# Other slots for the second element's spectra and for layer 2's weight sums in a two-layer kernel behind a Fourier filter

## The chip, the cores and the metric

The kernel runs on one core of a Trainium2 chip. The metric is the device time of one execution in microseconds, taken as the median of several runs. One further execution was profiled; all rows below come from it.

## What is computed

Each of two batch elements (3008 tokens of 256 channels) is filtered in the frequency domain, and the 6016 tokens then go through two feed-forward layers of width 2048. All of it is float32.

```
X = np.fft.rfft(x, axis=1)
y = np.fft.irfft(X * (filt_r + 1j * filt_i), n=3008, axis=1)
h = y.reshape(6016, 256) @ w_in
g = np.maximum(h, 0.0) + alpha * np.minimum(h, 0.0)
z = g @ w_out
h2 = np.maximum(z @ w2_in, 0.0)
out = (h2 * h2) @ w2_out
```

## The kernel before

The five engines each run a program written out by hand; semaphores join them, and each engine takes its instructions in the order in which they stand. TensorE (PE) does the matrix products, ScalarE (ACT) and VectorE (DVE) read PSUM, GpSimd (POOL) helps with SBUF to SBUF work, and SyncE (SP) issues nearly all DMAs.

A float32 product is made of three fast ones: each operand is cut into a high part (rounded) and a low part (the rest), and high by high, low by high and high by low are summed.

The first element's transform comes first, alone. Then runs a loop over **slots**, `n = 0 .. 191`. The tokens are cut into 12 groups of 500 or 504, and the hidden units into 8 pairs of 128-wide tiles, so a slot is one pair `p = n % 8` of one group `g = n // 8`; slots 0 to 95 are layer 1, the others layer 2. In slot n:

- PE runs `up(n)` (12 matmuls in two halves `j`, into one PSUM bank each), then `down_high(n - 2)` and `down_low(n - 2)` (21 matmuls of 250 columns: seven products in place of eight, by a Strassen scheme). In slots with `p = 2` the low part is put off to the middle of the next `up`.
- ACT writes the two ReLUs, `g_raw`, and later the high part `g_hi` of the slot before (L606).
- DVE turns each half into the activation with one operation (L913; both are one name, `g_raw`, and each adds one to `g_ready`), makes two sums (L923), and then `g_low(n - 1)`, the low part `g_lo` (L898). With `p = 1` the outputs of the group before are put together (`combine`, L883 to L892) and `g_low` is put off, so that DVE runs two of them in the slot with `p = 2`.
- POOL makes two more sums (L594, L597), after which ACT can write `g_hi`.

`up(n + 1)` of half j waits until DVE has done L913 of slot n, half j (`g_ready`), since it writes over the bank.

Into slots 0 to 95 work of two other kinds is put, by tables of slot numbers.

- **The second element's transform.** It has 12 units u. In slot `B_SLOT[u]` PE makes the spectrum (L1028 to L1031, three matmuls of 512 columns, `spectrum_1`) at the end of its slot; ACT swaps its halves (`swapped`) at the start of the next slot; DVE multiplies with the filter at the end of its own slot `B_SLOT[u]` (L805 `product_re`, and four pieces L812 `product_im`); POOL adds the two in the next slot (L560). Two slots on, ACT and POOL split the result into `y_hi` and `y_lo`, and four slots on (`V_LAG`) PE does the inverse (`inverse_1`, the same lines L1028 to L1031, before a spectrum that has the same slot). The product lives in one of two buffers, `slot = n % f.deep` with `deep` 2, and so unit u waits for the inverse of unit u - 2:

```
dve.wait_ge(f.v_done, free(n, f.deep))
```

- **Sums of layer 2's weights.** For each of the 8 pairs q, a load is issued in slot `W2_SLOT[q]`; in the next slot DVE makes four sums of 128x128 tiles (`sums`, L822 to L829) as the last thing of its slot; ACT (`s_hi`), POOL (`s_lo`, in three parts, three to five slots on) and two stores to HBM follow.

In slots with `p = 5` PE also makes the next group's input from the first element's or the second's transform (`y_group`, L1080), and waits there for the DVE products of all spectra that stand in slots before.

Of the kernel before, what the change touches and what calls it, by code (L numbers as in the profile page):

```python
# [75 lines left out]
AHEAD_BANK = (2, 3, 0, 1)  # L76
AHEAD_PART = (1, AHEAD_A - 2, AHEAD_A)
A_SLOT = [None] * AHEAD_A + [0, 1, 2, 2, 3, 3, 4, 4]
B_SLOT = [12, 14, 16, 20, 22, 24, 28, 30, 32, 34, 36, 38]
V_LAG = 4  # L80
CONST_SLOT = 7
VC_P, Y_P, IN_P = 3, 5, 6
LATE_W = 5
W2_SLOT = [45, 51, 57, 63, 69, 75, 81, 88]
W2_LOW = ((3, 0, 4), (4, 4, 8), (5, 8, W_T))

WARM_COLS, WARM_X = 2 * P, 8
# [98 lines left out]
def spectral_mix_two_ffn(nc, x, filt, w1, w2, alpha, sign, consts, consts_1, consts_full, const_y, out):  # L186
# [7 lines left out]
    with ctx:  # L194
# [95 lines left out]
        def _(sp):  # L290
# [50 lines left out]
            def load_filter(f, n, slot):  # L341
                if f is f1 or n >= f.filters:
                    sp.wait_ge(f.im_ready, free(n, f.filters))

                for c in ((n % 2,) if f is f0 else (0, 1)):
                    sp.dma_start(f.filt[c * N2:(c + 1) * N2, slot, :], filt[n * N2:(n + 1) * N2, :]
                                 ).then_inc(f.filt_loaded[slot], 16)

            def store_v(f, half, m, slot):
                sp.wait_ge(f.v_ready, done(half * B_HALF + m))  # L350
                sp.dma_start(v_rows[f.batch].rearrange("(p k) d -> p k d", k=K1)
                             [:, m * WIDE:(m + 1) * WIDE, half * P:(half + 1) * P],
                             f.v_out[:, slot, :].rearrange("p (k d) -> p k d", k=WIDE)
                             ).then_inc(f.v_stored[slot], 16)
# [86 lines left out]
            for n in range(2 * SLOTS_1):  # L441
# [6 lines left out]
                if n < SLOTS_1:  # L448
# [9 lines left out]
                    for u in range(B_UNITS):  # L458
                        if B_SLOT[u] - 3 == n:
                            if u == 0:  # L460
# [4 lines left out]
                    for u in range(B_UNITS):  # L465
                        if B_SLOT[u] - 1 == n:
                            load_filter(f1, u, u % f1.filters)
                    for u in range(B_UNITS):
                        if B_SLOT[u] + V_LAG + 1 == n:
                            store_v(f1, *divmod(u, B_HALF), u % f1.vs)  # L470
# [5 lines left out]
                for q in range(FP):  # L476
                    if W2_SLOT[q] + 6 == n:
                        cols = slice(q * W_T * P, (q + 1) * W_T * P)
# [6 lines left out]
                for q in range(FP):  # L485
                    if W2_SLOT[q] == n:
                        if q > 0:
# [40 lines left out]
        def _(pool):  # L528
# [27 lines left out]
            def add(n):  # L556
                slot = n % f1.deep
                pool.wait_ge(f1.re_ready, done(n))
                pool.wait_ge(f1.im_ready, done(n))
                pool.tensor_tensor(f1.y_re[:, slot, :], f1.y_re[:, slot, :], f1.y_im[:, slot, :],  # L560
                                   ALU.add).then_inc(f1.y_ready, 1)
# [4 lines left out]
            for n in range(2 * SLOTS_1):  # L566
                r, h = n % RING, HALF[n // FP % GROUPS]

                if n < SLOTS_1:
                    for u in range(B_UNITS):  # L570
                        if B_SLOT[u] + 1 == n:
                            add(u)
                    for u in range(B_UNITS):
                        if B_SLOT[u] - 1 == n:
                            pool.wait_ge(f1.t_hi_ready, u + 1)
                            low(f1.t_lo[:, u % f1.raw, :], f1.t_raw[:, u % f1.raw, :], f1.t_hi[:, u % f1.raw, :],
                                f1.t_lo_ready)
                        if B_SLOT[u] + 2 == n:
                            pool.wait_ge(f1.y_hi_ready, u + 1)
                            low(f1.y_lo[:, u % f1.deep, :], f1.y_re[:, u % f1.deep, :], f1.y_hi[:, u % f1.deep, :],  # L580
                                f1.y_lo_ready)
                    for q in range(FP):
                        for at, a, b in W2_LOW:
                            if W2_SLOT[q] + at == n:
                                pool.wait_ge(s_hi_ready, q + 1)
# [15 lines left out]
        def _(act):  # L601
# [100 lines left out]
            for n in range(2 * SLOTS_1):  # L702
# [54 lines left out]
                for q in range(FP):  # L757
                    if W2_SLOT[q] + 2 == n:
                        act.wait_ge(s_sums_ready, q + 1)
# [12 lines left out]
        def _(dve):  # L772
# [46 lines left out]
            def sums(raw, loaded, need, signal, at):  # L819

                dve.wait_ge(loaded, need)
                dve.scalar_tensor_tensor(out=raw[:, S1N, :], in0=raw[:, A21, :], scalar=-1.0, in1=raw[:, A22, :],  # L822
                                         op0=ALU.mult, op1=ALU.subtract).then_inc(signal[1], 1)
                dve.wait_ge(signal[1], 3 * at + 1)
                dve.scalar_tensor_tensor(out=raw[:, S2, :], in0=raw[:, S1N, :], scalar=-1.0, in1=raw[:, A11, :],
                                         op0=ALU.mult, op1=ALU.subtract).then_inc(signal[1], 1)
                dve.tensor_tensor(raw[:, S3, :], raw[:, A11, :], raw[:, A21, :], ALU.subtract).then_inc(signal[1], 1)
                dve.wait_ge(signal[1], 3 * at + 3)
                dve.tensor_tensor(raw[:, S4, :], raw[:, A12, :], raw[:, S2, :], ALU.subtract).then_inc(signal[0], 1)  # L829
# [72 lines left out]
            for n in range(2 * SLOTS_1):  # L902
# [43 lines left out]
                for q in range(FP):  # L946
                    if W2_SLOT[q] + 1 == n:
                        sums(s_raw, s_loaded, 16 * q + 16, (s_sums_ready, s_sum_step), q)
# [362 lines left out]
```

## Time and profile before

| what | value |
|---|---|
| median of 3 runs | 1121.08 us (1120.23 to 1121.08) |
| the profiled execution: its time, and its span from first to last instruction | 1121.51 us, 1119.7 us |
| PE busy | 1111.2 us, 99% |
| DVE busy | 961.2 us, 86% |
| ACT busy | 662.5 us, 59% |
| POOL busy | 650.4 us, 58% |
| share of PE in the chain that ended last | 88% (DVE 4%, all else 2% and less each) |
| the slots 0 to 95 | from 66.52 us to 614.73 us |

Busy time is the union of an engine's instructions. A matmul's end is modelled and overlaps the start of the next one, so the length of a slot is best read from the start of its first matmul (L1102) to that of the next slot's.

### The profile page before, as it was taken

Reading aid. Unit: us, or ns where it says so; the run is one execution under the profiler, and the core shown is the slowest. Engines: PE = TensorE matmul, PEld = TensorE weight load, DVE = VectorE, ACT = ScalarE, POOL = GpSimd, SP = SyncE. Lnnn points to the kernel's source line nnn. Section 1 sums busy time; section 2 is a strip of 40 time slices with the busy share of each in tenths; the row PEclk is TensorE's granted clock in tenths of the full one; section 3 lists DMA queues with packets and bytes.
Section 4 is the critical chain, followed back from the end, with each engine's and each line's share of the span. In section 5 each row is a group of like instructions: output and inputs, shape, how many; then the busy total and the mean of one; then the engine's idle time right before and its main releaser. Section 6 shows DMA issues by size and latency. Waiting matters only on the chain.

```text
span 1119.7 us, 17393 instructions
## 1 busy us (share of the span) xinstructions
PE 1111.2 (99%) x6997; PEld 992.1 (89%) x6997; DVE 961.2 (86%) x1099; ACT 662.5 (59%) x785; POOL 650.4 (58%) x479
## 2 busy tenths in 40 slices
PE   9999999999999999999999999999999999999998
PEld 8568999898999989999898999999999999999997
DVE  4748899989988998898988888888898898888887
ACT  4956566766655555555555565555556555555653
POOL 0837587777856567666657455455455555555453
PEclk9999999999999999999999999999999999999999
DMA  9973225144120431312318600110110110110100
GB/s 213 276 222 85 68 67 134 34 111 133 40 78 1 137 97 59 110 49 89 110 60 297 228 23 14 38 34 4 37 37 1 37 38 1 38 38 1 38 19 19
DMA packets 56408, 87.24 MB, mean 78 GB/s; under 512 B 4712, under 2 KB 44168, under 8 KB 56328
## 3 DMA queue, kind: packets, MB, share of 16 engines
q1 hardware_dynamic: 56128, 85.98, 26.2%
q8 instruction: 55, 0.90, 0.3%
q14 instruction: 25, 0.20, 0.1%
q10 hardware_dynamic: 200, 0.15, 0.0%
HBM read 52.82 MB, written 33.29 MB: 77 GB/s over the span
## 4 chain that ended last, share of the span: by engine, by line
PE 88%; DVE 4%; DMA 2%; ACT 2%; issue 1%; POOL 1%; SPq 1%; DVEq 0%; ACTq 0%; POOLq 0%
PE bank L1102 15%; PE bank L1107 15%; PE bank L1103 14%; PE bank L1141 13%; PE bank L1128 13%; PE bank L1130 13%; PE bank L1080 3%; DMA filt_b<-filt 2%; DVE g_lo L898 1%; DVE g_raw L913 1%; PE bank L1000 1%; ACT filt_b L606 1%; PE bank L994 1%; DMA vc<-v_rows 0%; ACT t_hi_b L606 0%
## 5 line engine op out<-in xcount | busy, mean ns | idle before, releaser
L594 POOL TENSOR_TENSOR g_raw<-g_raw 128x250 f32<-128x250 f32 (+1 forms) x191 | 280.9, 1471 | 393.4 <-DVE g_raw L923 393.4
L898 DVE TENSOR_TENSOR g_lo<-g_raw,g_hi 128x1750 fp32r<-128x1750 f32 (+1 forms) x191 | 424.0, 2220 | 45.1 <-ACT g_hi L606 44.4
L732 ACT ACTIVATE g_raw<-bank 128x500 f32<-128x500 f32 (+1 forms) x384 | 226.2, 591 | 320.5 <-PE bank L1107 280.9
L606 ACT ACTIVATE g_hi<-g_raw 128x1750 fp32r<-128x1750 f32 (+1 forms) x191 | 318.9, 1670 | 50.4 <-POOL g_raw L597 48.8
L1130 PE MATMUL bank<-g_hi,w_lo 128*128 128x250 f32 (+1 forms) x1337 | 320.0, 279 | 0.0
L1128 PE MATMUL bank<-g_hi,w_hi 128*128 128x250 f32 (+1 forms) x1337 | 319.5, 279 | 0.0
L1102 PE MATMUL bank<-in_hi,w_hi 128*128 128x500 f32 (+1 forms) x768 | 302.3, 394 | 2.0 <-DVE g_raw L913 2.0
L1103 PE MATMUL bank<-in_hi,w_lo 128*128 128x500 f32 (+1 forms) x768 | 298.3, 388 | 0.0
L1130 PEld LDWEIGHTS bank<-g_hi,w_lo 128*128 128x128 f32 x1337 | 252.8, 189 | 7.5
L1128 PEld LDWEIGHTS bank<-g_hi,w_hi 128*128 128x128 f32 x1337 | 252.5, 189 | 7.4
L597 POOL TENSOR_TENSOR g_raw<-g_raw 128x250 f32<-128x250 f32 (+1 forms) x191 | 247.8, 1297 | 15.0
L1107 PE MATMUL bank<-in_lo,w_hi 128*128 128x500 f32 (+1 forms) x768 | 236.8, 390 | 0.0
L1141 PE MATMUL bank<-g_lo,w_hi 128*128 128x250 f32 (+1 forms) x1337 | 187.7, 280 | 0.3
L1141 PEld LDWEIGHTS bank<-g_lo,w_hi 128*128 128x128 f32 x1337 | 171.3, 189 | 3.5 <-DVE g_lo L898 2.0
L1107 PEld LDWEIGHTS bank<-in_lo,w_hi 128*128 128x128 f32 x768 | 144.4, 188 | 30.1
L1102 PEld LDWEIGHTS bank<-in_hi,w_hi 128*128 128x128 f32 x768 | 144.6, 188 | 25.8 <-DVE g_raw L913 2.6
L1103 PEld LDWEIGHTS bank<-in_hi,w_lo 128*128 128x128 f32 x768 | 144.5, 188 | 23.5 <-issue 1.4
L913 DVE SCALAR_TENSOR_TENSOR g_raw<-g_raw,rest_sb,bank 128x500 f32<-128x500 f32 (+1 forms) x192 | 135.9, 729 | 33.1 <-ACT g_raw L732 33.1
L916 DVE TENSOR_TENSOR g_raw<-g_raw,bank 128x500 f32<-128x500 f32 (+1 forms) x192 | 127.7, 670 | 33.0 <-ACT g_raw L732 31.9
L923 DVE TENSOR_TENSOR g_raw<-g_raw 128x500 f32<-128x500 f32 (+1 forms) x192 | 135.5, 706 | 6.6
L1080 PEld LDWEIGHTS bank<-const_y_sb,vc 96*128 96x128 f32 x288 | 33.2, 192 | 1.7 <-DMA vc<-v_rows 1.6
L1080 PE MATMUL bank<-const_y_sb,vc 96*128 96x94 f32 (+4 forms) x288 | 33.7, 273 | 0.2 <-DMA vc<-v_rows 0.2
(87 smaller groups left out, 612.7 us busy)
## 6 DMA issues: line engine op xcount, KB each, us to landing
filt_b<-filt SPq DMA_DIRECT2D x36, 256.0 KB, 4.6
vc<-v_rows SPq DMA_DIRECT2D x22, 288.0 KB
v_rows<-v_out_b SPq DMA_DIRECT2D x24, 256.0 KB, 4.5
w_rows<-s_hi SPq DMA_DIRECT2D x8, 704.0 KB, 5.3
w_rows<-s_lo SPq DMA_DIRECT2D x8, 704.0 KB, 3.5
w_hi<-w_rows SPq DMA_DIRECT2D x8, 704.0 KB, 5.4
w_lo<-w_rows SPq DMA_DIRECT2D x8, 704.0 KB, 7.6
w_raw<-w SPq DMA_DIRECT2D x8, 512.0 KB, 8.7
```

The costliest lines, as they stand in the source:

```text
L594: pool.tensor_tensor(g_raw[:, r, T2, 0:h], g_raw[:, r, B22, 0:h], g_raw[:, r, T1N, 0:h], ALU.add).then_inc(t2_ready, 1)
L597: pool.tensor_tensor(g_raw[:, r, T4, 0:h], g_raw[:, r, B21, 0:h], g_raw[:, r, T2, 0:h], ALU.subtract).then_inc(t4_ready, 1)
L606: return act.activation(dst, src, ACT.Copy)
L732: act.activation(g_raw[:, r, 2 * j:2 * j + 2, 0:h], h_ps[j][:, 0:2 * h].rearrange("p (j d) -> p j d", j=2), ACT.Relu, scale=-1.0 if n < SL ...
L898: dve.tensor_tensor(g_lo[:, q, B11:T4 + 1, 0:h], g_raw[:, q, B11:T4 + 1, 0:h], g_hi[:, q, :, 0:h], ALU.subtract).then_inc(g_lo_ready, 1)
L913: dve.scalar_tensor_tensor(out=piece, in0=piece, scalar=rest_sb[:, f:f + 1], in1=hidden, op0=ALU.mult, op1=ALU.add).then_inc(g_ready, 1)
L1102: pe.matmul(o, w_hi[:, p, 2 * j + k, :], in_hi[:, g % 2, k, cols], start=(k == 0), stop=False)
L1103: pe.matmul(o, w_lo[:, p, 2 * j + k, :], in_hi[:, g % 2, k, cols], start=False, stop=False)
L1107: mm = pe.matmul(o, w_hi[:, p, 2 * j + k, :], in_lo[:, g % 2, k, cols], start=False, stop=(k == KD - 1))
L1128: pe.matmul(o, w_hi[:, p, tile, :], g_hi[:, q, piece - B11, 0:h], start=(first and side == 0), stop=False, skip_group_check=True)
L1130: pe.matmul(o, w_lo[:, p, tile, :], g_hi[:, q, piece - B11, 0:h], start=False, stop=False, skip_group_check=True)
L1141: mm = pe.matmul(o, w_hi[:, p, tile, :], g_lo[:, q, piece, 0:h], start=False, stop=last, skip_group_check=True)
```

## The change

Two tables of slot numbers get other values; nothing else is touched.

```diff
-B_SLOT = [12, 14, 16, 20, 22, 24, 28, 30, 32, 34, 36, 38]
+B_SLOT = [11, 12, 14, 16, 19, 20, 22, 24, 27, 28, 30, 32]
...
-W2_SLOT = [45, 51, 57, 63, 69, 75, 81, 88]
+W2_SLOT = [39, 46, 52, 58, 66, 74, 82, 88]
```

The spectra stood three to a group (p = 4, 6, 0) and at last at p = 2, 4, 6; they now stand four to a group, at p = 3, 4, 6, 0. The sums, one slot after `W2_SLOT`, stood at p = 6, 4, 2, 0, 6, 4, 2, 1 and now stand at p = 0, 7, 5, 3, 3, 3, 3, 1. The inverses, four slots after the spectra, stood in slots 16, 18, 20, 24, 26, 28, 32, 34, 36, 38, 40, 42 and now stand in 15, 16, 18, 20, 23, 24, 26, 28, 31, 32, 34, 36.

On PE, the first inverse before the change, at the end of slot 16, with unit 2's spectrum behind it (`L1028` with `y_hi` is an inverse, with `t_hi` a spectrum):

```order
L1141 MATMUL bank<-g_lo,w_hi 128x250 [waits g_lo_ready]
L1141 MATMUL bank<-g_lo,w_hi 128x250 x6
L1028 MATMUL bank<-y_hi_b,const_b 128x512 [waits y_hi_ready_b1,v_ready_b1,in_lo_ready]
L1029 MATMUL bank<-y_hi_b,const_b 128x512
L1031 MATMUL bank<-y_lo_b,const_b 128x512 [waits y_lo_ready_b1]
L1028 MATMUL bank<-t_hi_b,const_b 128x512 [waits t_hi_ready_b1,im_ready_b1,const_ready_b1,in_lo_ready]
L1029 MATMUL bank<-t_hi_b,const_b 128x512
L1031 MATMUL bank<-t_lo_b,const_b 128x512 [waits t_lo_ready_b1]
```

And the first inverse after the change, at the end of slot 15, with the first matmul of slot 16 behind it:

```order
L1141 MATMUL bank<-g_lo,w_hi 128x250 [waits g_lo_ready]
L1141 MATMUL bank<-g_lo,w_hi 128x250 x6
L1028 MATMUL bank<-y_hi_b,const_b 128x512 [waits y_hi_ready_b1,v_ready_b1,in_lo_ready]
L1029 MATMUL bank<-y_hi_b,const_b 128x512
L1031 MATMUL bank<-y_lo_b,const_b 128x512 [waits y_lo_ready_b1]
L1102 MATMUL bank<-in_hi,w_hi 128x500 [waits in_hi_ready,g_ready]
```

The inverse has moved up by one slot, and unit 2's spectrum by two, from the end of slot 16 to that of slot 14.

On DVE, the end of slot 14 and the start of slot 15, which read alike in both kernels but for their unit: before, the product (L805, L812) is that of unit 1; after the change it is that of unit 2, and its wait for `v_done_b1` is the one for unit 0's inverse. These are the rows after the change:

```order
L923 TENSOR_TENSOR g_raw<-g_raw 128x2x250 [waits g_ready]
L898 TENSOR_TENSOR g_lo<-g_raw,g_hi 128x7x250 [waits g_hi_ready]
L805 TENSOR_TENSOR y_re_b<-bank,filt_b 128x512 [waits filt_loaded0_b1,v_done_b1,swap_ready_b1,spec_done_b1]
L812 SCALAR_TENSOR_TENSOR y_im_b<-swapped_b,sign_sb,filt_b 128x128 x4
L913 SCALAR_TENSOR_TENSOR g_raw<-g_raw,rest_sb,bank 128x2x250 [waits relu_ready] x2
L923 TENSOR_TENSOR g_raw<-g_raw 128x2x250 [waits g_ready]
```

What moved is which unit stands there: slots 11 and 12 now hold units 0 and 1.

On DVE, slots 58 and 59 (p = 2 and 3) before the change, with the weight sums between them:

```order
L898 TENSOR_TENSOR g_lo<-g_raw,g_hi 128x7x250 [waits g_hi_ready]
L822 SCALAR_TENSOR_TENSOR s_raw<-s_raw 128x128 [waits s_loaded]
L825 SCALAR_TENSOR_TENSOR s_raw<-s_raw 128x128 [waits s_sum_step]
L827 TENSOR_TENSOR s_raw<-s_raw 128x128
L829 TENSOR_TENSOR s_raw<-s_raw 128x128 [waits s_sum_step]
L913 SCALAR_TENSOR_TENSOR g_raw<-g_raw,rest_sb,bank 128x2x250 [waits relu_ready] x2
```

And the same place after the change:

```order
L898 TENSOR_TENSOR g_lo<-g_raw,g_hi 128x7x250 [waits g_hi_ready]
L913 SCALAR_TENSOR_TENSOR g_raw<-g_raw,rest_sb,bank 128x2x250 [waits relu_ready] x2
L923 TENSOR_TENSOR g_raw<-g_raw 128x2x250 [waits g_ready]
L898 TENSOR_TENSOR g_lo<-g_raw,g_hi 128x7x250 [waits g_hi_ready]
L822 SCALAR_TENSOR_TENSOR s_raw<-s_raw 128x128 [waits s_loaded]
L825 SCALAR_TENSOR_TENSOR s_raw<-s_raw 128x128 [waits s_sum_step]
```

The sums have moved from the end of slot 58 to that of slot 59.

## Rows read from the trace of the kernel before

**Rows 1.** The page: the span, busy time, the granted PE clock by slices.

```profile
span 1119.7 us, 17393 instructions
...
PE 1111.2 (99%) x6997; PEld 992.1 (89%) x6997; DVE 961.2 (86%) x1099; ACT 662.5 (59%) x785; POOL 650.4 (58%) x479
...
PEclk9999999999999999999999999999999999999999
```

**Rows 2.** Waits of PE and its weight loads: us in total, times, longest.

```profile
PE bank L1102 <- DVE g_raw L913: 2.0, 3, 1.2
...
PEld bank L1141 <- DVE g_lo L898: 2.0, 6, 0.6
```

**Rows 3.** Timeline of PE, first matmuls of slots: start us, us, instruction, [idle before].

```profile
127.77 0.39 PE L1102 MATMUL bank<-in_hi,w_hi 128*128 128x500 f32 x1
...
133.78 0.39 PE L1102 MATMUL bank<-in_hi,w_hi 128*128 128x500 f32 x1
...
139.62 0.40 PE L1102 MATMUL bank<-in_hi,w_hi 128*128 128x500 f32 x1
...
153.07 0.39 PE L1031 MATMUL bank<-t_lo_b,const_b 128*128 128x512 f32 x1
153.29 0.39 PE L1102 MATMUL bank<-in_hi,w_hi 128*128 128x500 f32 x1
...
158.44 0.39 PE L1102 MATMUL bank<-in_hi,w_hi 128*128 128x500 f32 x1
...
165.00 0.39 PE L1102 MATMUL bank<-in_hi,w_hi 128*128 128x500 f32 x1
...
170.15 0.40 PE L1102 MATMUL bank<-in_hi,w_hi 128*128 128x500 f32 x1
...
272.32 0.39 PE L1102 MATMUL bank<-in_hi,w_hi 128*128 128x500 f32 x1
...
279.62 0.49 PE L1102 MATMUL bank<-in_hi,w_hi 128*128 128x500 f32 x1 [1.15 <-DVE g_raw L913]
...
416.65 0.50 PE L1102 MATMUL bank<-in_hi,w_hi 128*128 128x500 f32 x1 [0.42 <-DVE g_raw L913]
```

**Rows 4.** The chain that ended last, at the end of slot 35: start us, us, what.

```profile
277.40 1.52 DVE y_im_b L812 x4
278.92 0.66 DVE g_raw L913
```

**Rows 5.** Timeline of DVE, slots 12 to 17.

```profile
137.20 1.37 DVE L913 SCALAR_TENSOR_TENSOR g_raw<-g_raw,rest_sb,bank 128x500 f32<-128x500 f32 x2
...
141.86 0.68 DVE L805 TENSOR_TENSOR y_re_b<-bank,filt_b 128x512 f32<-128x512 f32 x1
142.46 1.12 DVE L812 SCALAR_TENSOR_TENSOR y_im_b<-swapped_b,sign_sb,filt_b 128x128 f32<-128x128 f32 x4
143.51 1.36 DVE L913 SCALAR_TENSOR_TENSOR g_raw<-g_raw,rest_sb,bank 128x500 f32<-128x500 f32 x2
...
154.79 0.69 DVE L805 TENSOR_TENSOR y_re_b<-bank,filt_b 128x512 f32<-128x512 f32 x1
155.40 1.61 DVE L812 SCALAR_TENSOR_TENSOR y_im_b<-swapped_b,sign_sb,filt_b 128x128 f32<-128x128 f32 x4
156.93 1.37 DVE L913 SCALAR_TENSOR_TENSOR g_raw<-g_raw,rest_sb,bank 128x500 f32<-128x500 f32 x2
...
165.14 2.56 DVE L898 TENSOR_TENSOR g_lo<-g_raw,g_hi 128x1750 fp32r<-128x1750 f32 x1 [1.14 <-ACT g_hi L606]
...
169.27 1.37 DVE L913 SCALAR_TENSOR_TENSOR g_raw<-g_raw,rest_sb,bank 128x500 f32<-128x500 f32 x2
```

**Rows 6.** Timeline of ACT, the swap behind a spectrum.

```profile
153.49 1.21 ACT L606 ACTIVATE swapped_b<-bank 64x512 f32<-64x512 f32 x2 [0.47 <-PE bank L1031]
```

**Rows 7.** The tile `s_raw`: instructions, ns min/median/max, first and last start.

```profile
L822 DVE SCALAR_TENSOR_TENSOR s_raw<-s_raw x8: 284/824/826, 348.2 to 585.7; 128x128 f32<-128x128 f32 x8
L825 DVE SCALAR_TENSOR_TENSOR s_raw<-s_raw x8: 291/774/775, 349.0 to 586.0; 128x128 f32<-128x128 f32 x8
```

## The prediction

> **What bounds the kernel now.** I read the busy times and the clock first, then the waits of TensorE, then the timelines of TensorE and VectorE slot by slot.
>
> TensorE is busy for 99% of the span, at the full granted clock in all 40 slices (2.4 GHz, the upper of its two levels); VectorE follows with 86% [rows 1]. So the time is TensorE's own work plus the few places where it has to wait. That work is the same after the change. What a table of slots can alter is the waits alone, and they are small now. TensorE waits three times for a VectorE activation (L913), 2.0 us together, and six times for a low part (L898), 2.0 us together by its weight loads [rows 2]; part of that second sum lies beside matmuls. A perfect table could take away about 4 us, 0.4%. There is much more room on the other side.
>
> The length of a slot is read from the starts of first matmuls [rows 3]. Slot 15 (p = 7, nothing added) goes from 153.29 to 158.44: 5.15 us. Slot 16, with an inverse and a spectrum, goes to 165.00: 6.56, so each of the two is worth 0.70. Slot 11 (p = 3, nothing added) takes 133.78 - 127.77 = 6.01; slot 35, with p = 3 and nothing added either, takes 279.62 - 272.32 = 7.30. The reader is to see in that last row that TensorE sat idle for 1.15 us, and whom it waited for.
>
> **Part 1: the spectrum at p = 2 goes (a gain).** The chain of work into slot 36 is four pieces of unit 9's product until 278.92, then an activation until 279.58, then the matmul at 279.62 [rows 3, 4]. Unit 9 stood in slot 34, p = 2, where VectorE has two low parts to make. No spectrum stands at p = 2 after the change. Gain: 7.30 - 6.01 = 1.3 us.
>
> **Part 2: a product now waits for an inverse that comes a slot later (the large term).** The product of unit u needs the buffer of unit u - 2, and that is free when TensorE has done the inverse of u - 2, four slots after its spectrum. In the old table `B_SLOT[u] - B_SLOT[u - 2]` is never under 4, and at 4 the inverse stands ahead of the spectrum in the same slot, so that the buffer is free by the time the spectrum is. In the new table it is 3 at three places: units 0 and 2 (slots 11, 14), units 4 and 6 (19, 22), units 8 and 10 (27, 30). There VectorE comes to the product at the end of its slot 14 (22, 30), and the inverse ends slot 15 (23, 31) of TensorE. Behind the blocked product stand, in order, both activations of slot 15, its sums and `g_low(14)`. TensorE can run all of slot 15 (what it needs was made ahead of the product), but the first matmul of slot 16 waits for the first activation of slot 15.
>
> How long does VectorE wait? In the trace it starts the product of slot 14 at 154.79, 1.5 us into slot 15 [rows 3, 5]; the inverse will end 5.15 + 0.70 = 5.85 us in. That is 4.3 us of VectorE, which it has no other use for. The price to TensorE is what follows the inverse before slot 16 may start:
>
> - the last matmul ends 0.17 us behind the moment at which the next one could have started: 153.07 + 0.39 = 153.46 against 153.29 [rows 3];
> - 0.03 us until a waiting engine starts: 153.49 by ScalarE behind that same matmul [rows 6];
> - product and first activation. In slot 13 they take from 141.86 to 143.51 + 0.73 = 144.24, 2.4 us; in slot 15, where GpSimd works beside them, from 154.79 to 156.93 + 0.73 = 157.66, 2.9 us [rows 5]. GpSimd will be idle at that moment, since its own next step waits for this product, so I take 2.4;
> - 0.04 us until TensorE starts, as at 279.62 [rows 3, 4].
>
> Together 2.6 us for each place, 3.1 with the longer product.
>
> Something follows. Before, the first activation of slot 15 was done at 157.66, 0.78 us ahead of slot 16 [rows 3, 5]; now it is 0.04 ahead. VectorE is thus 0.74 us later against TensorE than it is in the same slots today, and the work of slots 16 to 18 is the same in both kernels (inverse and spectrum in 16, an inverse in 18). The smallest margin that I find there is in slot 17: the activation from 169.27 ends at about 170.00, and TensorE starts slot 18 at 170.15 [rows 3, 5], 0.15 us. Against it stands an idle VectorE for 1.14 us ahead of the low part at 165.14 [rows 5], which takes up some of the delay, but not all, because ScalarE's high part, for which it waits, is late too. Bounds: 0 and 0.74 - 0.15 = 0.6; I take 0.4, nearer the upper one since that chain moves too. Each place costs 3.0, three of them **9.0 us** (7.2 to 11.1).
>
> **Part 3: spectra at p = 3 and in neighbouring slots (no cost taken).** Slots 11 and 12, 19 and 20, 27 and 28 now hold two spectra in a row. The cover is the margin of the activation in slot 12: it ends at 137.20 + 0.73 = 137.93, and slot 13 starts at 139.62 [rows 3, 5], 1.7 us ahead. A product adds 1.65 (141.86 to 143.51) to 2.1 (154.79 to 156.93) to VectorE, and the spectrum in slot 11 puts slot 12 off by 0.70, so 2.4 us stand against 1.65 to 2.1. The second product of the pair must be done before the input of the next group at p = 5 (L1080); I reckon its end as 0 to 1 us ahead of that. So 0, with up to 0.5 for each of three groups as a bound.
>
> **Part 4: the weight sums (a small loss).** Sums cost VectorE 1.1 us (the shortest of L822 and L825 and two short operations of 0.28) or, where GpSimd works beside them, 2.1 (the medians 0.82 and 0.77) [rows 7]. Two sets stood at p = 2 and brought two of the three waits: 2.0 - 1.15 = 0.85 together, one of them the 0.42 before 416.65 [rows 2, 3]. Those two go. Four sets now stand at p = 3 and delay the activation in the slot with p = 4. Without a spectrum, slot 12 would have ended at 139.62 - 0.70 = 138.92, so the margin is 138.92 - 137.93 = 1.0 us, against 1.1 to 2.1 of sums: 0.1 to 1.1 each, and I take 0.4, nearer the lower end, because what adds 0.5 to an operation is GpSimd's work, which at that place is blocked for only one of the two long ones. That is +1.6 - 0.85, and where p = 0 and 1 keep a set, the waits for low parts [rows 2] stay about as they are; 0.3 less for work that now stands in lighter slots at p = 5 and 7. Sum: **+0.5** (-1.0 to +2.5).
>
> **The sum.** Against the profiled execution, 1121.5 us (span 1119.7 and 1.8 around it), which is 0.4 above the median: -1.3 + 9.0 + 0 + 0.5 = +8.2. On the median: 1121.1 + 8.2 = **1129.3 us**. Lower bound: -1.3 + 7.2 - 1.0 = +4.9, 1126.0. Upper: -1.3 + 11.1 + 1.5 + 2.5 = +13.8, 1134.9.
>
> **A rule that would make it otherwise.** The clock is granted in full in all slices, one with an idle TensorE for 1.15 us among them [rows 1, 3]. The Trainium skill, page "TensorE: Matmul & The Clock Gate", part 1, says that the chip watches how busy TensorE has been and halves its clock after an idle stretch; by it waits of 2.6 us might do what those of 1.15 don't. No row here shows a fall, and the sum goes without it.
>
> **The rivals.**
>
> - *A fall of the clock.* Were each of the three waits followed by one slot at 1.2 GHz, each would cost another slot of 5.15 us: 1129.3 + 15.5 = 1144.8. The granted clock is against it [rows 1], the longer wait for it. Chance 0.03.
> - *Not slower: VectorE runs past the blocked product.* If the activations of slot 15, whose inputs are ready, went ahead of the product, each place would cost nothing, and parts 1 and 4 would remain: 1121.1 - 1.3 + 0.5 = 1120.3. It decides as soon as a place costs less than (1.3 - 0.5) / 3 = 0.27 us. Against it: at 165.14 VectorE stays idle for 1.14 us before a low part whose input is late [rows 5], and the order of rows is always that of the program. Chance 0.05, 0.03 of it over 0.2% faster.
> - *The change to the buffer's wait costs more than its own length.* VectorE stays late through p = 1 and 2, where outputs are put together and two low parts stand, and TensorE waits again in slots 17, 18 and 19, as it did in slot 35 with 1.3 us. Each place then costs 3.0 + 1.3 to 2.6, the whole comes to 1133 to 1137. Chance 0.12.
> - *It costs less.* Other work of slots 16 to 19 moves into the margins, the waits at p = 3 vanish and VectorE, rested, is never late again: each place 2.4, part 4 at -1.0: 1121.1 - 1.3 + 7.2 - 1.0 = 1126.0 or a little less. Chance 0.08.
>
> The forecast itself has 0.72.
>
> **The numbers.** What a measurement of this kernel can tell from no change is about 0.2%, 2.2 us. All cases but the second rival are slower by more: 0.95; that rival gives 0.03 faster and 0.02 the same. The range takes in the bounds of the terms, most of the cheaper rival and the lower end of the dearer one: 1125.5 to 1134.5.
>
> **What would show each step.** Part 2: in the waits, TensorE's L1102 on VectorE's L913 grows from 2.0 us in 3 to about 10 us, with three single waits of 2.4 to 2.9 us at the ends of slots 15, 23 and 31, and VectorE is idle for about 4 us before L805 there, released by TensorE's L1031; slot 15 lasts some 8.5 us. It is wrong if those waits are under 1 us or if VectorE's L913 of slot 15 starts before its L805. The 0.4 behind it: slots 16 and 17 together are 0 to 0.6 us longer than the 6.56 + 5.15 of now [rows 3]. Part 1: no idle TensorE at the end of a slot with p = 3 in groups with spectra, save small ones. Part 3: no wait of L1080 for a product. Part 4: small waits at the ends of slots 60, 68, 76 and 84, none at 59 and 83 of today's kind.

## The result, and the profile after

The changed kernel takes 1131.28 us (median of 6 runs, 1130.88 to 1132.73), the kernel before 1121.26 us (6 runs). The ratio is 1.009 with a 95% interval of 1.008 to 1.010: slower by 0.9%, 10 us. The profiled execution has a span of 1129.0 us, 9.3 more than before.

The waits of TensorE and its weight loads after the change, against [rows 2] (total us, times, longest), and one of VectorE's, which was not there before:

```profile
DVE y_re_b L805 <- PE bank L1031: 11.2, 3, 3.9
...
PEld bank L1102 <- DVE g_raw L913: 10.2, 5, 3.0
PE bank L1102 <- DVE g_raw L913: 8.5, 5, 2.6
...
PEld bank L1141 <- DVE g_lo L898: 2.8, 5, 1.1
...
PE bank L1141 <- DVE g_lo L898: 0.6, 1, 0.6
```

VectorE waits three times for an inverse (L1031) before a product (L805), and TensorE five times for an activation. Where these are is seen in the timeline of TensorE, the first matmuls of slots 15 to 18, 20, 24 and 32, against [rows 3]:

```profile
153.95 0.39 PE L1102 MATMUL bank<-in_hi,w_hi 128*128 128x500 f32 x1
162.51 0.49 PE L1102 MATMUL bank<-in_hi,w_hi 128*128 128x500 f32 x1 [2.58 <-DVE g_raw L913]
170.74 0.39 PE L1102 MATMUL bank<-in_hi,w_hi 128*128 128x500 f32 x1
175.89 0.39 PE L1102 MATMUL bank<-in_hi,w_hi 128*128 128x500 f32 x1
187.61 0.39 PE L1102 MATMUL bank<-in_hi,w_hi 128*128 128x500 f32 x1
216.46 0.50 PE L1102 MATMUL bank<-in_hi,w_hi 128*128 128x504 f32 x1 [2.58 <-DVE g_raw L913]
270.54 0.50 PE L1102 MATMUL bank<-in_hi,w_hi 128*128 128x500 f32 x1 [2.58 <-DVE g_raw L913]
```

Slot 15 lasts 162.51 - 153.95 = 8.56 us, and TensorE is idle for 2.58 at its end; the same 2.58 stands ahead of slots 24 and 32. The chain of work through the first of the three:

```profile
160.07 0.69 DVE y_re_b L805
160.77 1.05 DVE y_im_b L812 x4
161.81 0.66 DVE g_raw L913
162.47 0.04 issue
```

VectorE had been idle before that product for 3.56 us, as its timeline says:

```profile
160.07 0.69 DVE L805 TENSOR_TENSOR y_re_b<-bank,filt_b 128x512 f32<-128x512 f32 x1 [3.56 <-PE bank L1031]
```

Slot 16 is the surprise: 170.74 - 162.51 = 8.23 us with no wait in it, where the same work took 6.56 before [rows 3]. Four windows follow: the part of slot 16 with a lowered clock, the rest of that slot, and slots 24 and 32. Each line has the window and its length, the busy us of each engine, and then, as the third number from the end, the granted clock as a share of 2.4 GHz:

```profile
163.74:167.15 3.41, 3.41 (x11) 2.79 (x10) 3.41 (x3) 1.49 (x4) 3.41 (x2) 0.50 0.26 77
167.15:170.74 3.59, 3.59 (x26) 3.33 (x26) 3.47 (x4) 2.50 (x3) 2.90 (x4) 1.00 0.00 0
216.46:223.12 6.66, 6.66 (x39) 5.93 (x40) 6.25 (x6) 3.12 (x5) 6.58 (x5) 1.00 0.13 39
270.54:277.21 6.67, 6.67 (x40) 5.96 (x40) 6.27 (x6) 3.08 (x5) 6.59 (x5) 1.00 0.13 39
```

Behind the first of the three waits TensorE ran at 1.2 GHz for 3.41 us of slot 16; behind the other two it kept 2.4 GHz. The six runs of the changed kernel have mean clocks of 0.995 to 0.998, those of the kernel before 0.999 to 1.0, so each of the six had a fall somewhere.

### The profile page after: what moved, and what is told of

The parts are those of the page before. It is cut to its first block, busy times and chain, and to the rows that moved or that the text cites. A ratio compares the mean times of both kernels' runs of the same rounds, so it can differ in the third digit from the quotient of the medians.

```text
span 1129.0 us, 17393 instructions
## 1 busy us (share of the span) xinstructions
PE 1114.2 (99%) x6997; PEld 993.8 (88%) x6997; DVE 960.9 (85%) x1099; ACT 663.6 (59%) x785; POOL 646.2 (57%) x479
## 4 chain that ended last, share of the span: by engine, by line
PE 92%; DVE 3%; DMA 1%; POOL 1%; issue 1%; SPq 1%; ACT 1%; DVEq 0%; ACTq 0%; POOLq 0%
PE bank L1102 15%; PE bank L1107 15%; PE bank L1103 15%; PE bank L1141 13%; PE bank L1130 13%; PE bank L1128 13%; PE bank L1080 3%; DMA x_raw_b<-x 1%; PE bank L1023 1%; PE bank L1021 1%; DVE g_lo L898 1%; PE bank L994 1%; PE bank L1000 1%; DVE g_raw L913 1%; DVE y_im_b L812 0%
## 5 line engine op out<-in xcount | busy, mean ns | idle before, releaser
L594 POOL TENSOR_TENSOR g_raw<-g_raw 128x250 f32<-128x250 f32 (+1 forms) x191 | 269.3, 1410 | 397.8 <-DVE g_raw L923 397.8
L1102 PE MATMUL bank<-in_hi,w_hi 128*128 128x500 f32 (+1 forms) x768 | 302.9, 394 | 8.5 <-DVE g_raw L913 8.5
L597 POOL TENSOR_TENSOR g_raw<-g_raw 128x250 f32<-128x250 f32 (+1 forms) x191 | 249.8, 1308 | 15.0
L1107 PE MATMUL bank<-in_lo,w_hi 128*128 128x500 f32 (+1 forms) x768 | 237.4, 391 | 0.0
L1141 PE MATMUL bank<-g_lo,w_hi 128*128 128x250 f32 (+1 forms) x1337 | 187.8, 280 | 0.9 <-DVE g_lo L898 0.6
L1141 PEld LDWEIGHTS bank<-g_lo,w_hi 128*128 128x128 f32 x1337 | 171.3, 189 | 4.4 <-DVE g_lo L898 2.8
L1102 PEld LDWEIGHTS bank<-in_hi,w_hi 128*128 128x128 f32 x768 | 144.8, 189 | 33.5 <-DVE g_raw L913 10.2
L1107 PEld LDWEIGHTS bank<-in_lo,w_hi 128*128 128x128 f32 x768 | 144.7, 188 | 30.2
L923 DVE TENSOR_TENSOR g_raw<-g_raw 128x500 f32<-128x500 f32 (+1 forms) x192 | 139.2, 725 | 6.6
L1080 PEld LDWEIGHTS bank<-const_y_sb,vc 96*128 96x128 f32 x288 | 33.3, 192 | 1.3 <-DMA vc<-v_rows 0.8
L1080 PE MATMUL bank<-const_y_sb,vc 96*128 96x94 f32 (+4 forms) x288 | 33.7, 273 | 0.0
```

Source lines behind the costliest of these rows:

```text
L594: pool.tensor_tensor(g_raw[:, r, T2, 0:h], g_raw[:, r, B22, 0:h], g_raw[:, r, T1N, 0:h], ALU.add).then_inc(t2_ready, 1)
L597: pool.tensor_tensor(g_raw[:, r, T4, 0:h], g_raw[:, r, B21, 0:h], g_raw[:, r, T2, 0:h], ALU.subtract).then_inc(t4_ready, 1)
L1102: pe.matmul(o, w_hi[:, p, 2 * j + k, :], in_hi[:, g % 2, k, cols], start=(k == 0), stop=False)
L1107: mm = pe.matmul(o, w_hi[:, p, 2 * j + k, :], in_lo[:, g % 2, k, cols], start=False, stop=(k == KD - 1))
L1141: mm = pe.matmul(o, w_hi[:, p, tile, :], g_lo[:, q, piece, 0:h], start=False, stop=last, skip_group_check=True)
```

## The experiments

All are edits of the changed kernel but where said otherwise. The loop's slots are compared by their starts in the traces, since the time before slot 0 alone differs from one execution to the next (66.5 us before, 65.6 to 68.8 in the traces of the runs below). The ratio of each run is to executions of the kernel before that were taken together with it, with medians of 1121.56 to 1121.62 us.

**1. The inverse one slot earlier.**

```diff
-V_LAG = 4
+V_LAG = 3
```

> The changed kernel with V_LAG 3 in place of 4: every inverse stands one slot earlier, so units 2, 6 and 10 find their buffer free in the slot in which they are multiplied. The theory (the product waits for the inverse of the unit two before it, 2.7 us at three places, with a clock fall of 1.7 us and later waits of 2.3 us behind it) expects 1119 us, and no idle VectorE before L805. The rival (VectorE is overloaded by spectra at p = 3 and in neighbouring slots, wherever the inverse stands) expects no less than 1127.

Measured: 1121.21 us, ratio to the kernel before 0.9996 (0.9987 to 1.0005). The 10 us are gone, and so is VectorE's wait before L805. The floor that I expected, 1119, was not reached: slots 19 and 27, with a spectrum and an inverse each, last 8.80 and 8.51 us, 1.4 and 1.1 more than their own work (5.98 and 6.00 before, and 2 x 0.70). Run 2 shows why.

**2. A third buffer, nothing moved.**

```diff
-    f1 = Spectral(f1_scope, ctx, nc, "b1", 1, deep=2, ...
+    f1 = Spectral(f1_scope, ctx, nc, "b1", 1, deep=3, ...
```

> The changed kernel with three product buffers in place of two (deep = 3 for the second element), nothing moved. The product of unit u then waits for the inverse of unit u - 3, which is long done. The theory of the buffer expects 1119 us as with the earlier inverse; the rival of an overloaded VectorE expects 1127 or more; if it is the place of the inverse at p = 7 that costs, and not the wait, this one stays near 1131 while the earlier inverse helps.

Measured: 1121.55 us, 0.9998 (0.9988 to 1.0008). The inverses stand where they stood, at p = 7 too, and all of the loss is gone. So it is the buffer, and neither the place of the inverse nor the spectra at p = 3. (The buffer is more than the product: the program lays `y_lo` and `y_hi`, which the inverse reads, over the storage of `y_re` and `y_im`. That is why a product must wait for the inverse, and why `deep` gives all four a third place.) The last 2 us to my 1119 are in its waits, 1.3 us on TensorE and more on its weight loads:

```profile
PE bank L1141 <- DVE g_lo L898: 1.3, 2, 0.7
```

They stand in slots 19 and 27 (p = 3), which have a spectrum now. VectorE's and then GpSimd's timeline in slot 18 of this run:

```profile
175.80 3.07 DVE L898 TENSOR_TENSOR g_lo<-g_raw,g_hi 128x1750 fp32r<-128x1750 f32 x1
...
174.48 1.29 POOL L532 TENSOR_TENSOR y_lo_b<-y_re_b,y_hi_b 128x512 fp32r<-128x512 f32 x1
175.74 1.29 POOL L532 TENSOR_TENSOR t_lo_b<-t_raw_b,t_hi_b 128x512 fp32r<-128x512 f32 x1
```

In the kernel before the same low part took 1.98 us, with no `t_lo` beside it. A spectrum at p = 3 puts GpSimd's `t_lo` into the slot with p = 2, where VectorE makes two low parts; the first takes 3.07 us beside it, and slot 19 then lasts 7.63, against 5.98 + 0.70 = 6.68.

What decides is which of the two starts first, and the changed kernel itself shows both orders. These are its low part and `t_lo` in slot 18, and then in slot 26:

```profile
179.54 2.04 DVE L898 TENSOR_TENSOR g_lo<-g_raw,g_hi 128x1750 fp32r<-128x1750 f32 x1
179.70 3.04 POOL L532 TENSOR_TENSOR t_lo_b<-t_raw_b,t_hi_b 128x512 fp32r<-128x512 f32 x1
...
233.04 3.09 DVE L898 TENSOR_TENSOR g_lo<-g_raw,g_hi 128x1764 fp32r<-128x1764 f32 x1
232.99 1.29 POOL L532 TENSOR_TENSOR t_lo_b<-t_raw_b,t_hi_b 128x512 fp32r<-128x512 f32 x1
```

In slot 18 the low part is 0.16 us ahead, it is `t_lo` that lasts 3.04 us, and slot 19 loses nothing (6.69 us). In slot 26 `t_lo` is 0.05 us ahead, the low part lasts 3.09, and slot 27 lasts 7.60, 0.9 over 6.70. So slot 27 of the changed kernel loses 0.9 us that has nothing to do with the buffer: the third-buffer run has the same loss there (7.65).

**3. The new slots of the spectra alone, with the old `W2_SLOT`.**

> The new slots of the spectra with the old slots of the weight sums. By the slot lengths of the two traces the new sums gain 1.4 us, so this one should take 1132.7 us, 1.4 above the whole change. By the prediction's part 4 (new sums lose 0.5) it should take 1130.8.

Measured: 1134.07 us, 1.0106 (1.0091 to 1.0121), in the right direction for the gain of the sums but not separated by the intervals. The traces do separate it: slots 40 to 95 take 307.4 us here and 306.1 in the changed kernel, so the new sums gain 1.3 us. The rest of the difference between the two profiles is a longer fall of the clock behind the third wait of this execution, 6.83 us, of which this window shows the most; slots 31 to 35 take 34.30 us with it and 32.17 in the changed kernel. It had a fall behind the first wait too, and none behind the second:

```profile
270.20:276.70 6.50, 6.09 (x17) 5.08 (x18) 5.39 (x6) 2.40 (x5) 6.42 (x5) 0.50 0.13 40
```

**4. Four a group, but never closer than four slots to the unit two before.**

```diff
-B_SLOT = [11, 12, 14, 16, 19, 20, 22, 24, 27, 28, 30, 32]
+B_SLOT = [11, 12, 15, 16, 19, 20, 23, 24, 27, 28, 31, 32]
```

> The changed kernel with spectra at 11, 12, 15, 16, 19, 20, 23, 24, 27, 28, 31, 32: four to a group still, two neighbouring pairs, but unit u never closer than four slots to unit u - 2, so its buffer is free. The theory of the buffer expects 1119 to 1122 us. The rival of an overloaded VectorE, with two pairs a group in place of one, expects as much as the changed kernel, 1131 or more.

Measured: 1119.80 us, 0.9984 (0.9975 to 0.9993). Three edited numbers of the table take the 10 us away and leave the kernel with the lowest median of this study; the intervals of runs 7 and 9 overlap with its own.

**5. Is the price what stands behind the wait?** The product moved behind the first activation of the next slot, in one run for all twelve units, in another behind both.

```diff
                 for j in range(2):
                     ...
+                    if j == 0:
+                        for u in range(B_UNITS):
+                            if B_SLOT[u] + 1 == n:
+                                product_re(f1, u, ...)
+                                product_im(f1, u, ...)
...
-                        if B_SLOT[u] == n:
-                            product_re(f1, u, ...)
-                            product_im(f1, u, ...)
```

> The changed kernel, but VectorE takes each product one place later: behind the first activation of the next slot in place of ahead of it. The blocked product then holds back only the second activation, which TensorE needs 1.37 us into its slot. The theory (price = what stands behind the wait in VectorE's order) expects three waits of about 1.3 us in place of 2.6, no fall of the clock, and 1125.5 us. A rival in which TensorE pays for the late inverse itself expects no difference, 1131.

> As the run before, but the product stands behind both activations of the next slot. The theory expects the waits before L1102 to be gone, up to 1 us left before a low part (L1141) at each of the three places, full clock, and 1121 to 1123.5 us. The rival expects 1131.

Measured: 1136.98 us (1.0128, 1.0113 to 1.0144) and 1156.37 us (1.0301, 1.0285 to 1.0316). Both expectations missed by far. The three waits before L1102 were indeed 3.6 us together, 1.2 each, in the first, but nine other products were late too. TensorE waited before the next group's input, which needs them (L1080, 2.0 us in the first run and 10.6 in the second), and before low parts. The clock was not full either: it falls once in the first run's profile and three times in the second's. So I moved only the three blocked products (`u % 4 == 2`), again behind one and behind both activations.

> The changed kernel, with only the three blocked products (units 2, 6, 10) put behind the first activation of the next slot; the other nine stay where they are, unlike in the run that moved all twelve and lost time at the nine. Theory (price = what stands behind the wait): at each of the three places the wait before L1102 is 1.2 us in place of 2.6, but about 1 us comes before L1141, since the low part of slot 14 is still behind the product; no fall of the clock there; 1127 to 1129 us. A rival (TensorE pays for the late inverse itself): 1131.

> As the run before, behind both activations. Theory: no wait before L1102, 1.2 to 1.5 us before L1141 at each of the three places, full clock, 1124 to 1127 us. Rival: 1131.

Measured: 1131.15 us (1.0089, 1.0074 to 1.0104) and 1130.33 us (1.0078, 1.0063 to 1.0093). Both are the rival's 1131 and not what the theory said. In the first run the places of the waits came as expected. Its timeline of TensorE around slot 16:

```profile
162.62 0.50 PE L1107 MATMUL bank<-in_hi,w_hi 128*128 128x500 f32 x1 [1.22 <-DVE g_raw L913]
166.92 1.08 PE L1146 MATMUL bank<-g_lo,w_hi 128*128 128x250 f32 x7 [1.04 <-DVE g_lo L898]
174.91 0.49 PE L1107 MATMUL bank<-in_hi,w_hi 128*128 128x500 f32 x1 [0.38 <-DVE g_raw L913]
```

(Lines behind the edit are numbered 5 higher: L1107 is L1102, L1146 is L1141.) One wait of 2.6 has become 1.2 before the first matmul, 1.0 before the low part and 0.4 a slot later. In the second run the places did not come as expected. I had foreseen no wait before the first matmul of a slot; it came at the start of slots 18, 26 and 34, and another came before the inverse at the end of slots 16, 24 and 32 (L1033 here):

```profile
PE bank L1033 <- issue: 3.7, 3, 1.3
PE bank L1107 <- DVE g_raw L913: 3.7, 3, 1.3
```

The sums over five slots, from the starts of slots 15, 23 and 31 to those of 20, 28 and 36, say it best:

| kernel | slots 15 to 19 | 23 to 27 | 31 to 35 |
|---|---|---|---|
| changed | 33.67 us | 33.73 | 32.17 |
| three products behind the first activation | 33.66 | 33.58 | 32.10 |
| three products behind both | 33.54 | 33.58 | 32.01 |
| third buffer | 30.49 | 30.34 | 28.74 |

Wherever the wait is put, it costs 3.1 to 3.4 us a place against the same table without it. A reason can be read in the third-buffer run, slots 15 to 19 (busy us of TensorE, its weight loads, VectorE, ScalarE and GpSimd):

```profile
153.88:184.36 30.48, 29.78 (x181) 26.32 (x180) 28.87 (x35) 20.51 (x29) 23.53 (x18) 1.00 0.24 69
```

VectorE is busy for 28.87 of 30.48 us there, 95%, far more than its mean of 86%. It has no room to make up for 3.56 us of idleness. Behind both activations, VectorE stands still before the product for 1.8 us and then for 2.8, because ScalarE's next activation is behind work that waits for the same product:

```profile
160.41 0.69 DVE L805 TENSOR_TENSOR y_re_b<-bank,filt_b 128x512 f32<-128x512 f32 x1 [1.84 <-PE bank L1036]
...
167.44 1.38 DVE L913 SCALAR_TENSOR_TENSOR g_raw<-g_raw,rest_sb,bank 128x500 f32<-128x500 f32 x2 [2.80 <-ACT g_raw L732]
```

**6. The wait made longer.** For units 2, 6 and 10 the four pieces L812 are made twice, which leaves the result as it is.

> The changed kernel with the four pieces of the product's second half made twice for units 2, 6 and 10, behind the wait, 1.1 to 1.2 us more each. The theory expects each of TensorE's three waits to grow from 2.6 to 3.7 us, 3.4 us in all, 1134.7 us, and more falls of the clock than the changed kernel has: 1.7 to 3.4 us for each further place, up to 1141. If the clock falls for another reason than the idle TensorE, the mean clock stays at 0.998 to 0.995 and the time at 1134.7.

Measured: 1138.16 us, 1.0139 (1.0123 to 1.0155), mean clocks of 0.992 to 0.995. The wait, and three windows of the granted clock (lines numbered 11 higher):

```profile
PE bank L1113 <- DVE g_raw L924: 11.2, 3, 3.8
```

```profile
163.87:170.70 6.83, 5.44 (x14) 4.42 (x15) 6.29 (x8) 1.74 (x4) 5.91 (x4) 0.50 0.12 38
221.89:225.30 3.41, 3.41 (x10) 2.69 (x9) 3.41 (x2) 1.71 (x3) 3.41 (x3) 0.50 0.26 77
276.50:279.90 3.40, 3.35 (x8) 2.75 (x9) 3.37 (x3) 1.56 (x3) 3.40 (x3) 0.50 0.14 44
```

The time lies in the range expected with further falls (1134.7 to 1141). Waits of 3.75 us brought a fall to half the clock at all three places, as did the waits of 3.20 to 3.69 us before L1080 in the profile of run 5 that has all products behind both activations. Waits of 2.58 brought one at one of three places in the changed kernel's profile and at two of three in run 3's. At the places where run 5 split the wait into pieces of 1.3 us or less there was none. So a longer idle stretch brings the fall more often. But its length is not all: the first kernel of run 5 had a fall of 3.41 us at 204.60, in slot 21, behind an idle stretch of 0.83 us and the 24 short matmuls of L1080 (94 columns).

**7. No spectrum at p = 0.** Three buffers, and the fourth spectrum of a group at p = 7.

```diff
-B_SLOT = [11, 12, 14, 16, 19, 20, 22, 24, 27, 28, 30, 32]
+B_SLOT = [11, 12, 14, 15, 19, 20, 22, 23, 27, 28, 30, 31]
```

> Three product buffers, and the spectra at p = 3, 4, 6, 7 in place of 3, 4, 6, 0 (slots 11, 12, 14, 15, 19, 20, 22, 23, 27, 28, 30, 31). With three buffers alone two waits of about 0.95 us were left in slots 19 and 27 before L1141, behind a low part of 3.07 us. The theory that VectorE is still late there from the product at p = 0, which meets the sums of the outputs at p = 1, expects both to go: 1.9 us less than with three buffers, 1119.6. If only GpSimd's low part of the next group's first unit at p = 2 makes that low part long, they stay: 1121.5.

Measured: 1120.43 us, 0.9987 (0.9978 to 0.9997), between the two expectations. Slots 19 and 27 last 7.92 and 7.96 us, but they now hold an inverse too (the spectra of slots 15 and 23 have theirs there), so their own work is 7.38 and 7.40: 0.5 to 0.6 is lost in each, where it was 0.95. The waits shrank and did not go. The low part in slot 18 takes 2.86 us in place of 3.07; it starts 0.28 us behind `t_lo` in place of 0.06. `t_lo` at p = 2 is still what makes it long, and the move changed only by how much the two overlap.

**8. Other slots for the sums, on top of run 7.**

```diff
-W2_SLOT = [39, 46, 52, 58, 66, 74, 82, 88]
+W2_SLOT = [38, 44, 50, 58, 66, 74, 82, 90]
```

> The kernel with three product buffers and spectra at p = 3, 4, 6, 7, and the weight sums at p = 7, 5, 3, 3, 3, 3, 3, 3 (W2_SLOT 38, 44, 50, 58, 66, 74, 82, 90) in place of 0, 7, 5, 3, 3, 3, 3, 1. The slot lengths show sums at p = 0 and 1 to cost 0.4 us each and those at p = 3 nothing: 0.8 us less than with the sums of the change, 1119.6. Prediction's part 4 (0.4 us for each set at p = 3) would give 0.3 to 0.8 us more instead.

Measured: 1121.38 us, 0.9997 (0.9988 to 1.0007). Slots 43 and 91 gave back 0.2 and 0.4, slots 52 and 95 lost 0.9 each, for two different reasons. GpSimd's `s_lo` of the last set now stands beside the cut of layer 2's first input in slot 94 (L862), which takes 2.33 us; without it the two instructions took 1.26. And the sums in slot 51 wait for their load, which was issued in slot 50:

```profile
376.23 0.29 DVE L822 SCALAR_TENSOR_TENSOR s_raw<-s_raw 128x128 f32<-128x128 f32 x1 [0.90 <-DMA s_raw<-w]
```

**9. An even table.** Three buffers, `V_LAG = 3`, and both tables anew.

```diff
-B_SLOT = [11, 12, 14, 16, 19, 20, 22, 24, 27, 28, 30, 32]
+B_SLOT = [12, 14, 15, 20, 22, 23, 28, 30, 31, 36, 38, 39]
...
-W2_SLOT = [39, 46, 52, 58, 66, 74, 82, 88]
+W2_SLOT = [44, 50, 56, 62, 68, 74, 82, 90]
```

> A version that should leave hardly any wait: three product buffers, inverses three slots behind, spectra at 12, 14, 15, 20, 22, 23, 28, 30, 31, 36, 38, 39 (p = 4, 6, 7 alone) and sums at p = 5, 3, 1, 7, 5, 3, 3, 3. Before, slots 34 to 37 lost 1.5 us and the sums 2.2; here one set at p = 1 (0.4) and one at p = 7 (0.1) are left: 3.2 us less than the kernel before, 1118.3 us. If four spectra a group are not what costs the 2 us left with three buffers, it stays at 1120 or more.

Measured: 1120.22 us, 0.9990 (0.9980 to 0.9999). With no spectrum at p = 3, slots 19, 27 and 35 last 5.98, 6.00 and 5.99 us: every wait of the transform is gone, and slot 18's first low part takes 1.98 us. No `t_lo` stands at p = 2 in this table, so this agrees with what runs 2 and 7 say of it. What was gained there went into the sums (0.9 in slots 52 and 95, by the two causes of run 8, and 0.4 in slot 59).

## Why the prediction was right

**Part 2, the wait for the buffer, was right in mechanism and size.** 2.6 us a place were forecast, 2.58 came, three times; slot 15 was to last 8.5 and lasted 8.56. VectorE's idle time was put at 4 us and was 3.56 to 3.9. The chain has the steps of the sum: 0.69, 1.05, 0.66 and 0.04. Runs 1, 2 and 4 take the wait away in three ways and each takes away all 10 us. (The lower bound of 7.2 for this part was never worked out: three times 2.6 is 7.8.)

**What follows the wait had the right size, and a fall of the clock came on top.** I added 0.4 for each place, 1.2 in all. In the profile of the changed kernel nothing follows in slots 17 and 18 of the first place; in slots 24 to 26 there are 0.7 us, in slots 32 and 33 0.7: 1.4 in all. The fall of the clock added 1.7 in slot 16, a term that I had put at nothing. My sign for this step, slots 16 and 17 together 0 to 0.6 us longer, was therefore missed there (1.7) and hardly met at the other two places (slots 24 and 25, 32 and 33: 0.6 and 0.7). Slot 27 has 0.9 more, but that is part 3 and not the wait.

All told a place costs 3.1 to 3.4 us against the same table with three buffers, where I had 3.0. A place with a fall of 3.41 us (33.67) and one without a fall (33.73) are equally long, but by different parts: the first has the 1.7 of the clock, the second the 0.7 behind the wait and the 0.9 of slot 27. A fall is not free: the one of 6.83 us in run 3 made its place 2.1 us longer. That VectorE's lost time is the price fits the sums over five slots and VectorE's 95% there; it is not shown to the tenth of a microsecond. The reason that I gave, "product plus first activation" before TensorE may start, is how the price shows and not what sets it: with that order changed it stayed the same (run 5), as the rival of run 5 had said.

**Part 1 held:** slot 35 lasts 5.99 us in place of 7.30, 1.3 us as forecast.

**Part 3, no cost for spectra at p = 3, was wrong.** Slot 27 loses 0.9 in the changed kernel; slot 19 escapes because its low part happens to start 0.16 us ahead of `t_lo`. With the wait gone, both lose 0.95 (run 2). I looked at VectorE's own margin at p = 4 and not at what GpSimd must do a slot earlier.

**Part 4 had the wrong sign.** +0.5 was forecast; it is -1.3 (run 3). The step that failed is the 0.4 for each set at p = 3: 1.6 was forecast for the four, and nothing measurable came; none of the small waits that I named at the ends of slots 60, 68, 76 and 84 is there. And the two sets that left p = 2 had cost 1.4 (slots 59, 60, 83 and 84), not 0.85. VectorE's timeline at slot 59 (after the change):

```profile
428.24 2.33 DVE L898 TENSOR_TENSOR g_lo<-g_raw,g_hi 128x1750 fp32r<-128x1750 f32 x1 [1.14 <-ACT g_hi L606]
430.49 0.28 DVE L822 SCALAR_TENSOR_TENSOR s_raw<-s_raw 128x128 f32<-128x128 f32 x1
430.81 0.29 DVE L825 SCALAR_TENSOR_TENSOR s_raw<-s_raw 128x128 f32<-128x128 f32 x1
431.02 0.28 DVE L827 TENSOR_TENSOR s_raw<-s_raw 128x128 f32<-128x128 f32 x1
431.33 0.29 DVE L829 TENSOR_TENSOR s_raw<-s_raw 128x128 f32<-128x128 f32 x1
431.54 1.37 DVE L913 SCALAR_TENSOR_TENSOR g_raw<-g_raw,rest_sb,bank 128x500 f32<-128x500 f32 x2
```

The four sums take 1.05 us, the low end of 1.1 to 2.1, and the activation ends in time: slots 59 and 60 last 6.01 and 5.16 us.

**The sum.** By the slots of the profile: waits 3 x 2.73 = 8.2 (slot 15: 8.56 - 5.15 - 0.69 for the inverse, and its like), the clock 1.7, what follows the waits 1.4, slot 27 0.9, slots 35 to 37 -1.5, the sums -1.3: 9.4, against 9.3 in the spans. The forecast was 8.2. It had 0.4 too little for the waits, 1.7 for the clock, 0.2 for what follows and 0.9 for part 3, and 0.2 and 1.8 too much for parts 1 and 4. That the error of part 4 makes up for most of the missing clock and part 3 is luck. The large term is not, and with part 4 alone put right the forecast would have been 1127.5, still in the range. The medians lie 10.0 us apart, 0.7 more than the two profiled executions.

**The rival of the clock** had a chance of 0.03 and came true in part: at one of three places in the profile, and somewhere in each run. Its price was far under the 5.15 us that I gave it: 1.7 us in slot 16. With the rule of the Trainium skill, page "TensorE: Matmul & The Clock Gate", part 1, which I weighed and left out of the sum, the trace now agrees at one of the three places: the clock halves behind an idle stretch of 2.58 us and comes back.

What stays open: which stretch of 2.58 us brings a fall and which doesn't.

## What to carry to other kernels

In a table of slots, look first at the distance between a producer and the unit that last used its buffer, and then at what stands behind the waiting instruction in that engine's order: one slot too few at three places cost 10 us, where the best table of these runs gains 1.8. Look at how busy the second engine is in just those slots (95% here, 86% over the span): it stood still for 3.6 to 3.9 us at each place, and TensorE lost 3.2 to 3.4; with the wait put elsewhere in VectorE's order TensorE still lost 3.1 to 3.4. Another buffer or an inverse one slot earlier removed it, another order didn't. And count for each moved step the helper work that it drags one or two slots ahead, on the engine that slows the critical one when both work at once.

## What the hardware showed that I had not expected

A single idle stretch of 2.58 us was enough for TensorE's granted clock to fall from 2.4 to 1.2 GHz at three of six places in two profiles; 3.20 to 3.75 us did it at all six in two others. One fall came behind only 0.83 us of idleness and 24 short matmuls.

Between a VectorE instruction (`g_lo`, 128x1750, two inputs in SBUF) and a GpSimd one (`t_lo`, 128x512) the one that started first kept its time, 2.04 or 1.29 us, and the other lasted 3.04 or 3.07 us, though they started within 0.2 us of each other. A difference of 0.2 us in the starts thus moved 0.9 us from the engine with room to the one without.
